# Expert weights loaded from a list of used experts, with experts alternating large and small

## The chip, the cores and the metric

The kernel runs on one core of one Trainium2 chip. The metric is the device time of one execution in microseconds, smaller is better. TensorE (PE in the profile) does the matmuls, VectorE (DVE), ScalarE (ACT) and GpSimd (POOL) the rest, and SyncE (SP) issues most of the transfers. Each engine runs its own program in order and waits on semaphores.

## What is computed

Linear attention (4 batches, 576 tokens, 8 heads of 64), a mixer layer over tokens and channels, and then a layer of experts. Only the last concerns the change. Its core, for the token row `x[b, s]`:

```python
fresh_e = int(np.argmax(logits[b, s]))
if s == 0 or local_gate[b, s] < 0.5:
    e = fresh_e
else:
    e = prev_e if prev_e >= 0 else fresh_e
...
h = np.maximum(x[b, s] @ w1[e], 0.0)
out[b, s] = p[e] * (h @ w2[e])
```

There are 8 experts (`E`), each with `w1[e]` of 512x1024 and `w2[e]` of 1024x512 in float32, 4 MB together. How many tokens fall on an expert depends on the data. Evaluating the reference on this input gives, for experts 0 to 7, 0, 0, 0, 835, 973, 5, 88 and 403 tokens, which is 7, 8, 1, 1 and 4 tiles of 128 rows for experts 3 to 7, 21 tiles in all. In the first three batches alone the counts of experts 3 to 7 are 809, 806, 2, 88 and 23.

## The kernel before

**Stages.** The first part (attention and mixer) goes batch by batch. While the last batch is in its 32 channel chunks, `route_early(idx)` does small pieces of the routing of the first three batches between chunks: at `idx == 13` the counts of the experts are in `bank[3]`, and `order_experts` picks the expert with the most tokens (`expert0`). The others follow it cyclically by number (`expert_at`). Its weights are loaded at once, and the first `EARLY = 3` tiles are filled from the first three batches. The full routing of all tokens (`slots_of_lanes` and what follows) runs on DVE beside tiles 0 to 2. `ids` (row numbers of the tokens of each tile) and `table` (expert, version and so on of each tile) come out of it.

**A tile.** For tile t, POOL gathers 128 token rows into `xg` (`gather`), PE transposes them (`x_turn`), computes the hidden layer in two halves of 512 (`hidden`), transposes it (`h_turn`), multiplies by `w2` (`output`), DVE scales it (`yo_out`), and POOL scatters the rows to the output. PE's order within tile t from tile 3 on is:

```python
h_turn(t, 0, again)
hidden(t, n, 1, again)
x_turn(t + 1)
output(t, n, 0, again)
h_turn(t, 1, again)
next_n = version_of(t + 1)
hidden(t + 1, next_n, 0, again=True)
output(t, n, 1, again)
```

Each float32 weight is split into a high and a low part: ACT writes the high part, DVE the low part, both reading `w1raw` or `w2raw`. A set of weights has 8 units of 512 KB: 0 to 3 are `w1`, 4 to 7 are `w2`. The raw buffer holds one set, the split form two (slots `n & 1`). A set is called a version: version n is the n-th expert loaded.

**When weights are split.** `plan_loads` writes `plan`: an expert's second tile splits `w1` of the next version, its third tile splits `w2` of it; an expert with only one tile has to do both in that tile. For the first expert, tile 3 counts as the second tile. ACT and DVE do the splits between their other work of the tile, in program order.

**When weights are loaded.** SP waits for `routed >= 2` (tables and row numbers both written), then walks over the tiles from 1 on. For each it loads `table` entries into registers (lines 449, 439, 440), and where the tile begins a new expert it loads the 8 units, each behind a wait that the previous version's unit is split (`w_split`). The last of the eight positions counts as a change even if no tile belongs to it (`is_last`), so a set is also loaded behind the last tile.

Of the kernel before, what the change touches and what calls it, by code (L numbers as in the profile page):

```python
# [22 lines left out]
ALU = mybir.AluOpType  # L23
# [6 lines left out]
P = 128  # L30
# [6 lines left out]
def build(nc, q, k, v, w_tok1, w_tok2, w_ch1, w_ch2, w_gate, w_local, w1, w2, out):  # L37
# [42 lines left out]
    with ExitStack() as ctx:  # L80
# [14 lines left out]
        is_last = sb(ctx, "is_last", [1, E])  # L95
# [4 lines left out]
        expert_at = sb(ctx, "expert_at", [P, 2, E], I32)  # L100
        code_at = sb(ctx, "code_at", [P, E])
        token = sb(ctx, "token", [P, J])
# [45 lines left out]
        with ExitStack() as part2:  # L148
# [24 lines left out]
            table = sb(part2, "table", [1, 5, NTP], I32)  # L173
# [34 lines left out]
            expf = sb(part2, "expf", [1, NTP + 1])  # L208
            expert0 = sb(part2, "expert0", [1, 1])
            changes = sb(part2, "changes", [1, NTP + 1])  # L210
# [5 lines left out]
            tg = sb(part2, "tg", [1, NTP, E - 1])  # L216
            tw = sb(part2, "tw", [1, NTP, E - 1])
            starts = sb(part2, "starts", [1, E])
            expi = sb(part2, "expi", [1, NTP], I32)
# [32 lines left out]
        xg_cleared, order_known = sem("xg_cleared"), sem("order_known")  # L252
        own_counted, counts_ready, sel_counted, base_ready = sem("own_counted"), sem("counts_ready"), sem("sel_counted"), sem("base_ready")
# [73 lines left out]
        def _(sp):  # L327
# [92 lines left out]
            e = sp.value_load(expert_at[0:1, 1, 0:1], min_val=0, max_val=E - 1)  # L420
# [17 lines left out]
            def load_weights(t):  # L438
                e = sp.value_load(table[0:1, 0, bass.ds(t, 1)], min_val=0, max_val=E - 1)
                changed = sp.value_load(table[0:1, 1, bass.ds(t, 1)], min_val=0, max_val=1)  # L440
                with sp.If(changed):
                    before = sp.value_load(table[0:1, 4, bass.ds(t, 1)], min_val=0, max_val=E)
# [12 lines left out]
        def _(pe):  # L455
# [267 lines left out]
            def version_of(t):  # L723
                return pe.value_load(table[0:1, 2, bass.ds(t, 1)], min_val=0, max_val=E)
# [68 lines left out]
            with pe.Fori(EARLY, NT) as t:  # L793
                live = pe.value_load(table[0:1, 3, bass.ds(t + 1, 1)], min_val=0, max_val=1)
                with pe.If(live):
                    tile(t, again=True)
# [3 lines left out]
        def _(act):  # L800
# [219 lines left out]
            with act.Fori(EARLY, NT) as t:  # L1020
                live = act.value_load(table[0:1, 3, bass.ds(t + 1, 1)], min_val=0, max_val=1)
                with act.If(live):
                    tile(t, again=True)
# [3 lines left out]
        def _(dve):  # L1027
# [105 lines left out]
            def clear_routing():  # L1133

                beside(dve.memset(expf[:, 0:1], 0.0))
                beside(dve.memset(changes[:, 0:1], 0.0))
# [73 lines left out]
            def order_experts():  # L1210

                assert E & (E - 1) == 0
# [477 lines left out]
```

## Time and profile before

| | us |
|---|---|
| median of 3 runs | 794.91 (794.33 to 796.45) |
| profiled execution, its own time | 790.27 |
| its span in the profile | 788.6 |
| PE busy in the span | 749.5 (95%) |

The times that follow are read from the profiled execution, from the start of its span. Its first part lasts to about 487 us, the tiles of the experts fill the rest. A tile can be followed by PE's rows: L641 is `x_turn`, L718 `output`, L705 `h_turn`, L693 `hidden`. The start of `output(t, 0)` of tile t stands at 539.14 us for tile 3, 560.27 for 4, 609.73 for 8, 622.10 for 9, 696.29 for 15, 712.93 for 16, 729.80 for 17 and 742.39 for 18. The distance between two such starts is called a pitch here.

### The profile page before, as it was taken

What the parts mean: (1) busy time and instruction counts of PE and PEld (TensorE: products, weight loads), DVE (VectorE), ACT (ScalarE), POOL (GpSimd) and SP (SyncE); (2) the same over time, 40 slices, a digit from 0 to 9 for tenths busy, and PEclk for the clock granted to TensorE, in tenths of its full rate; (3) what the DMA queues carried; (4) which work ended last, traced back from release to release, by engine and by line L of the source; (5) the groups of instructions that cost most, each with busy time, mean ns of one, the idle gap of its engine ahead of it and who ended that gap; (6) DMA issues with size and microseconds to landing.
All of it is one profiled execution on the core that took longest, in us unless ns stands there. A gap on an engine that the chain in (4) does not pass through costs nothing.

```text
span 788.6 us, 14829 instructions
## 1 busy us (share of the span) xinstructions
PE 749.5 (95%) x4836; PEld 678.5 (86%) x4837; DVE 316.6 (40%) x611; ACT 234.1 (30%) x409; POOL 142.4 (18%) x162
## 2 busy tenths in 40 slices
PE   6999999999999999999999999996999999997993
PEld 6879999999999999999999999874888888875882
DVE  6746241225332235332225424762522622257450
ACT  3743042023132023133021141313422522255340
POOL 6562020002020002020000023111221221211220
PEclk9999999999999999999999999999999999999998
DMA  9932122012131012100010510105360620136400
GB/s 210 378 66 59 33 68 54 1 32 61 31 81 41 1 32 62 31 21 11 1 35 1 196 62 16 62 28 190 118 230 34 211 90 26 36 134 210 155 27 2
DMA packets 69514, 61.80 MB, mean 78 GB/s; under 512 B 51484, under 2 KB 53244, under 8 KB 69472
## 3 DMA queue, kind: packets, MB, share of 16 engines
q1 hardware_dynamic: 65952, 51.77, 22.2%
q0 software_dynamic: 3520, 9.44, 3.5%
q8 instruction: 30, 0.49, 0.3%
q14 instruction: 12, 0.10, 0.0%
HBM read 52.99 MB, written 10.31 MB: 80 GB/s over the span
## 4 chain that ended last, share of the span: by engine, by line
PE 80%; DVE 6%; issue 3%; DMA 3%; POOL 2%; ACT 2%; SPq 2%; DVEq 1%; ACTq 0%; POOLq 0%
PE bank L572 36%; PE bank L718 13%; PE bank L693 12%; PE bank L514 5%; PE bank L543 4%; POOL qb L1577 2%; PE bank L705 2%; PE bank L537 2%; PE bank L486 2%; DMA x_rows<-x1n 1%; PE bank L593 1%; PE bank L502 1%; PE bank L582 1%; PE bank L524 1%; PE bank L641 1%
## 5 line engine op out<-in xcount | busy, mean ns | idle before, releaser
L572 PE MATMUL bank<-u_h,wc_h 128*128 128x288 f32 x384 | 120.0, 312 | 1.5 <-DVE hid_l L1303 1.5
L718 PE MATMUL bank<-wslots,hT_h 128*128 (+1 forms) x336 | 107.5, 401 | 10.1 <-DVE hT_l L1470 10.1
L572 PE MATMUL bank<-hid_h,wc_h 128*128 128x288 f32 x384 | 117.0, 305 | 0.0
L693 PE MATMUL bank<-wslots,xgT_h 128*128 (+1 forms) x344 | 111.8, 406 | 4.2 <-DVE wslots L1454 3.1
L572 PE MATMUL bank<-hid_l,wc_h 128*128 128x288 f32 x384 | 113.2, 295 | 0.0
L572 PE MATMUL bank<-u_l,wc_h 128*128 128x288 f32 x384 | 113.1, 295 | 0.0
L572 PE MATMUL bank<-u_h,wc_l 128*128 128x288 f32 x384 | 113.0, 294 | 0.0
L572 PE MATMUL bank<-hid_h,wc_l 128*128 128x288 f32 x384 | 113.0, 294 | 0.0
L1303 DVE SCALAR_TENSOR_TENSOR hid_l<-bank,hid_h 128x288 fp32r<-128x288 f32 x96 | 43.3, 454 | 132.4 <-ACT hid_h L872 132.2
L718 PEld LDWEIGHTS bank<-wslots,hT_h 128*128 128x128 f32 x336 | 62.1, 191 | 23.5 <-issue 10.8
L693 PEld LDWEIGHTS bank<-wslots,xgT_h 128*128 128x128 f32 x344 | 61.0, 188 | 17.9 <-issue 7.0
L872 ACT ACTIVATE hid_h<-bank 128x288 fp32r<-128x288 f32 x96 | 38.9, 408 | 123.4 <-PE bank L572 123.4
L572 PEld LDWEIGHTS bank<-u_h,wc_h 128*128 128x128 f32 x384 | 72.1, 188 | 2.9 <-DVE hid_l L1303 1.8
L572 PEld LDWEIGHTS bank<-u_l,wc_h 128*128 128x128 f32 x384 | 72.2, 188 | 0.7
L572 PEld LDWEIGHTS bank<-hid_l,wc_h 128*128 128x128 f32 x384 | 72.2, 188 | 0.5
L572 PEld LDWEIGHTS bank<-hid_h,wc_h 128*128 128x128 f32 x384 | 72.0, 188 | 0.6
L572 PEld LDWEIGHTS bank<-hid_h,wc_l 128*128 128x128 f32 x384 | 72.3, 188 | 0.0
L572 PEld LDWEIGHTS bank<-u_h,wc_l 128*128 128x128 f32 x384 | 72.0, 188 | 0.0
L693 PE MATMUL bank<-wslots,xgT_l 128*128 (+1 forms) x172 | 67.4, 392 | 0.0
L718 PE MATMUL bank<-wslots,hT_l 128*128 (+1 forms) x168 | 66.3, 394 | 0.0
L1310 DVE TENSOR_TENSOR x1T<-bank,u_h 128x288 f32<-128x288 f32 x32 | 14.6, 457 | 117.2 <-PE bank L572 117.2
L1577 POOL TENSOR_TENSOR qb<-qb,qmax 96x768 f32<-96x768 f32 x12 | 17.6, 1471 | 231.2 <-DVE qmax L1072 231.2
(236 smaller groups left out, 1090.2 us busy)
## 6 DMA issues: line engine op xcount, KB each, us to landing
w1raw<-in_moe_w_dram SPq DMA_DIRECT2D x24, 512.0 KB, 4.6
w2raw<-in_moe_w_dram SPq DMA_DIRECT2D x24, 512.0 KB, 6.4
wc_raw<-in_moe_w_ch_dram SPq DMA_DIRECT2D x8, 768.0 KB, 11.2
x_rows<-x1n SPq DMA_DIRECT2D x24, 192.0 KB, 2.1
kb<-in_k_dram SPq DMA_DIRECT2D x24, 144.0 KB, 3.1
qb<-in_q_dram SPq DMA_DIRECT2D x24, 144.0 KB, 3.1
vb_e<-in_v_dram SPq DMA_DIRECT2D x16, 144.0 KB, 3.6
vb_o<-in_v_dram SPq DMA_DIRECT2D x16, 144.0 KB, 3.4
```

The source lines that it names most:

```text
L486: last = pe.matmul(k_bank(n, g)[:, c * KV:(c + 1) * KV], keys(n)[:, i, c * P:(c + 1) * P], vb[g][:, 2 * c:2 * c + 2, i, :], start=(i == 0) ...
L514: last = pe.matmul(mix_bank(n, g)[:, c * TOK:(c + 1) * TOK], queries(n)[:, i, c * P:(c + 1) * P], wt1[:, i, :], start=(i == 0), stop=(i == ...
L537: pe.matmul(bank[4 + j % 2][:, 0:HS], kvd[:, c // CG, c % CG, :], qT[:, c // CG, c % CG, part], start=True, stop=False)
L543: last = pe.matmul(bank[4 + j % 2][:, 0:HS], h1T[:, m, c * P:(c + 1) * P], wt2[:, m, part], start=False, stop=(m == KT - 1))
L572: last = pe.matmul(to, lhsT, rhs, start=(m == 0), stop=(m == len(mms) - 1))
L693: last = pe.matmul(bank[half][:, :], xgT[a][:, c, :], w1s[x][:, bass.ds(n & 1, 1), c, half * 512:(half + 1) * 512].rearrange("p a n -> p ( ...
L705: last = pe.transpose(bank[2 + half][:, c * P:(c + 1) * P], hs[:, f * P:(f + 1) * P], ident[:, :])
L718: last = pe.matmul(bank[5][:, :], hT[a][:, f, :], w2s[x][:, bass.ds(n & 1, 1), f, :].rearrange("p a n -> p (a n)"), start=(f == 0 and (a, ...
L872: act.activation(hid[0][:, i, :], bank[idx % 2][:, 0:HS], ACT.Relu).then_inc(hid_hi, 1)
L1303: dve.scalar_tensor_tensor(out=hid[1][:, i, :], in0=psum, scalar=0.0, in1=hid[0][:, i, :], op0=ALU.max, op1=ALU.subtract).then_inc(chan_do ...
L1310: dve.tensor_tensor(x1T[:, i, :], psum, u[0][:, i, part], ALU.add).then_inc(y_sum, 1)
L1577: pool.tensor_tensor(by_head(queries(n))[:, IHALF[part], :, :], x[:, IHALF[part], :, :], by[:, IHALF[part], :].unsqueeze(3).broadcast_to([ ...
```

## The change

Three things are done. (1) `order_experts` only finds the first expert; a new `place_experts`, run on DVE at `idx == 15`, ranks all experts by their count in the first three batches and places ranks 0, 1, 2, ... of the asked-for experts alternately from the large and the small end. (2) A new `versions`, on DVE ahead of `yo_out(1)`, writes a list `loads` of the experts that have tiles; SP waits for it (`versions_known`) and loads set after set from the list, with no walk over tiles and no set for an expert without tiles. (3) On DVE `ids_out` comes ahead of `tables`; POOL waits only for the row numbers before it gathers tile 3; PE does the first half of `output(2, ..., 1)` ahead of `x_turn(3)`.

```diff
             def order_experts():
-                then(dve.tensor_scalar(expert_at[:, 0, :], lane[:, 0:E], top0[:, E + 1:E + 2], float(E), ALU.subtract, ALU.add))
-                then(dve.tensor_scalar(expert_at[:, 1, :], expert_at[:, 0, :], E - 1, None, ALU.bitwise_and))
-                beside(dve.tensor_copy(expert0[:, :], expert_at[0:1, 1, 0:1]))
-                then(dve.tensor_scalar(code_at[:, :], expert_at[:, 1, :], -1.0, float(E), ALU.mult, ALU.add), order_known)
+                then(dve.tensor_scalar(expert0[:, :], top0[0:1, E + 1:E + 2], -1.0, float(E), ALU.mult, ALU.add), order_known)
+
+            def place_experts():
+
+                beside(dve.scalar_tensor_tensor(out=key[:, :], in0=bank[3][:, 0:E], scalar=float(E), in1=code[:, :], op0=ALU.mult, op1=ALU.add))
+                then(dve.tensor_scalar(asked[:, :], bank[3][:, 0:E], 0.0, None, ALU.is_gt))
+                beside(dve.tensor_reduce(twice[:, 0:1], asked[:, :], AX_X, ALU.add))
...
+                then(dve.tensor_reduce(rank[:, :], over_key[:, :, :], AX_X, ALU.add))
+                then(dve.tensor_scalar(up[:, :], rank[:, :], 2.0, None, ALU.mult))
+                then(dve.scalar_tensor_tensor(out=down[:, :], in0=up[:, :], scalar=-1.0, in1=twice[:, 1:2].broadcast_to([P, E]), op0=ALU.mult, op1=ALU.add))
+                beside(dve.scalar_tensor_tensor(out=place[:, :], in0=down[:, :], scalar=0.0, in1=rank[:, :], op0=ALU.is_lt, op1=ALU.mult))
+                then(dve.tensor_tensor(up[:, :], up[:, :], down[:, :], ALU.min))
+                then(dve.tensor_tensor(place[:, :], place[:, :], up[:, :], ALU.max))
...
@@ SP @@
-            sp.wait_ge(routed, 2)
-            with sp.Fori(1, NT + 1) as t:
-                go = sp.value_load(table[0:1, 3, bass.ds(t, 1)], min_val=0, max_val=1)
-                with sp.If(go):
-                    load_weights(t)
+            def load_weights(n):
+
+                e = sp.value_load(loads[0:1, 0, n:n + 1], min_val=0, max_val=E - 1)
+                asked_for = sp.value_load(loads[0:1, 1, n:n + 1], min_val=0, max_val=1)
+                with sp.If(asked_for):
                     for i in range(NU):
-                        sp.wait_ge(w_split, NU * before + i + 1)
+                        sp.wait_ge(w_split, NU * (n - 1) + i + 1)
                         load_unit(e, i)
+            sp.wait_ge(versions_known, 1)
+            for n in range(1, E):
+                load_weights(n)
@@ PE @@
             output(2, 0, 0, True, SECOND)
+            output(2, 0, 1, True, FIRST)
             x_turn(EARLY)
-            output(2, 0, 1, True)
-            pe.wait_ge(routed, 1)
+            output(2, 0, 1, True, SECOND)
+            pe.wait_ge(routed, 2)
@@ DVE @@
             row_lanes(P, rowhot, rows_hot)
+            versions()
             yo_out(1, True)
 
             hT_out(2, 0)
+            ids_out()
             tables()
-            ids_out()
             plan_loads()
@@ POOL @@
-                    pool.wait_ge(routed, 2)
+                    pool.wait_ge(routed, 1)
```

`versions` is nine small operations on one partition (the last writes `loads` and signals `versions_known`); `tables` has 7 in place of 13.

On SP, behind its last stores of token rows, stood the walk over tiles. These are its first rows, one pass up to the branch that skips a tile without a new expert; the loads of the units follow that branch:

```order
L448 UNCONDITIONAL_BRANCH [waits routed]
L448 ISA
L449 TENSOR_LOAD table
L449 ISA x2
L450 COMPARE_AND_BRANCH
L439 ISA
L439 TENSOR_LOAD table
L439 ISA x2
L440 ISA
L440 TENSOR_LOAD table
L440 ISA x2
L441 COMPARE_AND_BRANCH
```

At the same place of SP now stands the first entry of the list, with the first unit of the weights right behind it:

```order
L451 TENSOR_LOAD loads [waits versions_known]
L451 ISA x2
L452 TENSOR_LOAD loads
L452 ISA x2
L453 COMPARE_AND_BRANCH
L381 ISA [waits w_split]
L381 DMA w1raw<-in_moe_w_dram 128x1024
```

The walk is gone: two register loads stand between the wait and the first transfer, where each pass of the walk has three.

On DVE, beside tile 2, the end of `tables` (L1409 to L1417) stood ahead of the row numbers `ids` (`ids_out`, L1422 to L1424); `yo_out(1)` and `hT_out(2, 0)` stand ahead of both:

```order
L1409 CAST tiles<-first_tile 1x1
L1411 TENSOR_SCALAR expi<-expf,expert 1x29
L1412 TENSOR_SCALAR table<-expi 1x29 [waits route]
L1413 CAST table<-changes 1x29
L1414 CAST table<-changes 1x29
L1415 TENSOR_TENSOR changed<-expf 1x29
L1416 TENSOR_SCALAR table<-lane,first_tile 1x29
L1417 CAST table<-changed 1x29 [waits route]
L1422 COPY prob_t<-bank 128x24 [waits ids_ready,route,routed]
L1423 TENSOR_SCALAR ids<-bank 128x24
L1424 TENSOR_TENSOR prob_t<-prob_t,bank 128x24 [waits route,routed]
```

Now the end of `versions` (L1438, L1439) comes ahead of `yo_out(1)` (L1514), and the row numbers ahead of `tables` (L1443 on):

```order
L1438 TENSOR_REDUCE loads_f<-by_version 1x8 [waits route]
L1439 CAST loads<-loads_f 1x8 [waits route]
L1514 TENSOR_SCALAR yo<-bank,prob_t 128x512 [waits y_ready,rows_stored,route,versions_known]
L1503 TENSOR_TENSOR hT_l<-bank,hT_h 128x512 [waits hT_hi]
L1455 COPY prob_t<-bank 128x24 [waits ids_ready]
L1456 TENSOR_SCALAR ids<-bank 128x24
L1457 TENSOR_TENSOR prob_t<-prob_t,bank 128x24 [waits route,routed]
L1443 TENSOR_TENSOR tg<-lane,first_tile 1x232 [waits route]
L1446 TENSOR_REDUCE begun<-tg 1x29 [waits route]
```

`ids` moved ahead of the tables, and the nine operations of `versions` ahead of the scaling of tile 1.

On PE, at the end of tile 2, `x_turn(3)` (L641) stood between the two halves of `output(2)`:

```order
L718 MATMUL bank<-wslots,hT_h 128x512 x2
L718 MATMUL bank<-wslots,hT_l 128x512
L641 MATMUL bank<-ident,xg 128x128 [waits x_in]
L641 MATMUL bank<-ident,xg 128x128 x3
L718 MATMUL bank<-wslots,hT_h 128x512 [waits w_split,hT_done]
L718 MATMUL bank<-wslots,hT_h 128x512
```

Now six matmuls of the second half stand ahead of it:

```order
L727 MATMUL bank<-wslots,hT_h 128x512 [waits w_split,hT_done]
L727 MATMUL bank<-wslots,hT_h 128x512
L727 MATMUL bank<-wslots,hT_l 128x512
L727 MATMUL bank<-wslots,hT_h 128x512 x2
L727 MATMUL bank<-wslots,hT_l 128x512
L650 MATMUL bank<-ident,xg 128x128 [waits x_in]
L650 MATMUL bank<-ident,xg 128x128 x3
```

PE's wait for the gathered rows (`x_in`) moved behind those six.

## Rows read from the trace of the kernel before

**Rows 1.** Stretches: length, busy of PE, PEld, DVE, ACT, POOL, granted clock, DMA share, GB/s.
```profile
539.14:560.27 21.13, 14.48 (x64) 11.56 (x63) 7.45 (x8) 7.03 (x10) 2.44 (x4) 0.84 0.60 214
...
609.73:622.10 12.37, 12.37 (x62) 10.19 (x61) 7.46 (x8) 6.68 (x10) 3.15 (x4) 1.00 0.63 213
...
696.29:712.93 16.64, 13.50 (x61) 9.72 (x60) 11.91 (x12) 11.96 (x17) 2.12 (x3) 1.00 0.63 219
712.93:729.80 16.87, 13.46 (x61) 9.96 (x61) 11.90 (x12) 9.40 (x13) 3.06 (x4) 1.00 0.57 190
729.80:742.39 12.59, 12.59 (x61) 10.47 (x62) 2.82 (x4) 2.20 (x4) 3.49 (x5) 1.00 0.56 216
```

**Rows 2.** Timeline of PE in tile 3: start, length, instruction, idle before and its releaser.
```profile
551.99 1.22 PE L718 MATMUL bank<-wslots,hT_h 128*128 x2 [6.65 <-DVE hT_l L1470]
```

**Rows 3.** The chain that ended last, in order of time: start, length, what.
```profile
524.08 0.29 SPq L449
...
542.47 0.37 SPq L370
543.12 5.41 DMA w1raw<-in_moe_w_dram
...
551.99 4.64 PE bank L718 x12
...
560.27 2.77 PE bank L718 x12
```

**Rows 4.** Timeline of DVE beside tiles 1 and 2.
```profile
516.21 2.69 DVE L1202 TENSOR_TENSOR rowhot<-sloti,lane 128x768 fp32r<-128x768 int32 x3
519.40 0.75 DVE L1481 TENSOR_SCALAR yo<-bank,prob_t 128x512 f32<-128x512 f32 x1 [0.51 <-PE bank L718]
...
521.07 0.14 DVE L1403 SCALAR_TENSOR_TENSOR starts<-ntl,is_last 1x8 f32<-1x8 f32 x1
...
523.40 0.17 DVE L1417 CAST table<-changed 1x29 int32<-1x29 f32 x1
...
523.71 0.17 DVE L1423 TENSOR_SCALAR ids<-bank 128x24 int32<-128x24 f32 x1
```

**Rows 5.** Timeline of POOL, PE and DVE around x_turn(3).
```profile
525.16 1.06 POOL L1613 DMA_INDIRECT xg<-x_rows,id_in  x1 [0.87 <-POOL id_in L1610]
...
528.65 0.66 PE L641 MATMUL bank<-ident,xg 128*128 128x128 f32 x4 [0.88 <-DMA xg<-x_rows,id_in]
...
529.98 0.69 DVE L1294 TENSOR_TENSOR xgT_l<-bank,xgT_h 128x512 fp32r<-128x512 f32 x1 [2.14 <-ACT xgT_h L909]
...
531.88 0.61 PE L693 MATMUL bank<-wslots,xgT_h 128*128 x2
```

**Rows 6.** DMA issues between 570 and 576 us: count, KB, median us to landing.
```profile
out_dram<-yo,id_out POOLq DMA_INDIRECT x1, 7.5
xg<-x_rows,id_in POOLq DMA_INDIRECT x1, 6.0
```

**Rows 7.** DMA issues between 445 and 452 us.
```profile
xg<-x_rows,id_in POOLq DMA_INDIRECT x1, 7.6
```

**Rows 8.** Timeline of DVE and PE behind chunk 15 of the last batch.
```profile
442.55 0.46 DVE L1303 SCALAR_TENSOR_TENSOR hid_l<-bank,hid_h 128x288 fp32r<-128x288 f32 x1 [0.57 <-ACT hid_h L872]
...
447.88 0.38 PE L572 MATMUL bank<-u_h,wc_h 128*128 128x288 f32 x1
```

**Rows 9.** Timeline of SP and POOL around those transfers.
```profile
446.97 1.92 SPq L374 DMA_DIRECT2D w2raw<-in_moe_w_dram  x4
448.76 1.23 POOL L1613 DMA_INDIRECT xg<-x_rows,id_in  x1 [0.98 <-POOL id_in L1610]
...
568.38 2.10 SPq L370 DMA_DIRECT2D w1raw<-in_moe_w_dram  x4
570.67 2.77 SPq L374 DMA_DIRECT2D w2raw<-in_moe_w_dram  x4
```

**Rows 10.** The stretch in which the later of those two sets landed, columns as in Rows 1.
```profile
568.38:583.00 14.62, 14.62 (x73) 12.07 (x72) 3.79 (x6) 3.48 (x6) 2.44 (x4) 1.00 0.90 322
```

More of the change, by code:

```diff
@@ L99, in build @@
         top0 = sb(ctx, "top0", [P, E + 2])
-        expert_at = sb(ctx, "expert_at", [P, 2, E], I32)
+        expert_at = sb(ctx, "expert_at", [P, E])
+        expert0 = sb(ctx, "expert0", [1, 1], I32)
         code_at = sb(ctx, "code_at", [P, E])
+        key = sb(ctx, "key", [P, E])
+        over_key = sb(ctx, "over_key", [P, E, E])
+        rank = sb(ctx, "rank", [P, E])
+        asked = sb(ctx, "asked", [P, E])
+        twice = sb(ctx, "twice", [P, 2])
+        up = sb(ctx, "up", [P, E])
+        down = sb(ctx, "down", [P, E])
+        place = sb(ctx, "place", [P, E])
         token = sb(ctx, "token", [P, J])
@@ L170, in build @@
             id_out = sb(part2, "id_out", [P, 1], I32)
[L173 removed]
+            table = sb(part2, "table", [1, 2, NTP], I32)
             plan = sb(part2, "plan", [1, 4, NTP], I32)
@@ L215, in build @@
             slots = sb(part2, "slots", [P, J, E])
[L216 to L219, printed above, removed]
+            tg = sb(part2, "tg", [1, NTP, E])
+            used = sb(part2, "used", [1, E])
+            used_before = sb(part2, "used_before", [1, E + 1, E])
+            version_at = sb(part2, "version_at", [1, E + 1])
+            named = sb(part2, "named", [1, E])
+            by_version = sb(part2, "by_version", [1, E, E])
+            loads_f = sb(part2, "loads_f", [1, E])
+            loads = sb(part2, "loads", [1, 2, E], I32)
             yo = sb(part2, "yo", [P, D])
@@ L252, in build @@
         xg_cleared, order_known = sem("xg_cleared"), sem("order_known")
+        versions_known = sem("versions_known")
         own_counted, counts_ready, sel_counted, base_ready = sem("own_counted"), sem("counts_ready"), sem("sel_counted"), sem("base_ready")
@@ L419, in _ @@
             sp.wait_ge(order_known, 1)
-            e = sp.value_load(expert_at[0:1, 1, 0:1], min_val=0, max_val=E - 1)
+            e = sp.value_load(expert0[0:1, 0:1], min_val=0, max_val=E - 1)
             for i in range(FU):
@@ L1286, in route_early @@
                     early_lanes()
+                elif idx == 15:
+                    place_experts()
                 elif idx == 17:
@@ new lines, in versions @@
+            def versions():
+                then(dve.tensor_scalar(used[:, :], ntl[0:1, :], 0.0, None, ALU.is_gt))
+                beside(dve.tensor_tensor(used_before[:, :, :], used[:, :].unsqueeze(1).broadcast_to([1, E + 1, E]), below[0:1, :, :], ALU.mult))
+                then(dve.tensor_tensor(named[:, :], used[:, :], expert_at[0:1, :], ALU.mult))
+                then(dve.tensor_reduce(version_at[:, :], used_before[:, :, :], AX_X, ALU.add))
+                beside(dve.tensor_scalar(loads[:, 1, :], lane[0:1, 0:E], version_at[:, E:E + 1], None, ALU.is_lt))
+                then(dve.tensor_tensor(by_version[:, :, :], version_at[:, 0:E].unsqueeze(1).broadcast_to([1, E, E]),
+                                       lane[0:1, 0:E].unsqueeze(2).broadcast_to([1, E, E]), ALU.is_equal))
+                then(dve.tensor_tensor(by_version[:, :, :], by_version[:, :, :], named[:, :].unsqueeze(1).broadcast_to([1, E, E]), ALU.mult))
+                then(dve.tensor_reduce(loads_f[:, :], by_version[:, :, :], AX_X, ALU.add))
+                then(dve.tensor_copy(loads[:, 0, :], loads_f[:, :]), versions_known)
@@ L1433, in plan_loads @@
                 beside(dve.tensor_tensor(only, now, ahead, ALU.mult))
-                beside(dve.tensor_scalar(more, changes[:, 1:NTP + 1], changes[:, NTP:NTP + 1], None, ALU.is_lt))
-                then(dve.tensor_scalar(plan[:, 3, :], changes[:, 1:NTP + 1], 1.0, None, ALU.add))
+                beside(dve.tensor_scalar(more, begun[:, 1:NTP + 1], begun[:, NTP:NTP + 1], None, ALU.is_lt))
+                then(dve.tensor_copy(plan[:, 3, :], begun[:, 1:NTP + 1]))
                 beside(dve.scalar_tensor_tensor(out=later, in0=now, scalar=0.0, in1=more, op0=ALU.is_equal, op1=ALU.mult))
```

55 lines of the change are left out of this document (23 added, 32 removed).

## Prediction

> **What bounds the kernel now.** I read the page first: PE is busy 95% of the span, so only places where PE stands still can give time back, or places where it would newly stand still. The change touches the stage of the experts, so next I cut that stage at each start of `output(t, 0)` and read the pitches [rows 1]. An undisturbed tile takes 12.37 us, and that includes a tile in which ACT and DVE split the four `w1` units of the next expert: the stretch of tile 8 has 7.46 us of DVE work and PE is still busy for all of its 12.37 [rows 1]. So a split costs nothing if its raw weights are there. Three stretches are longer, and one slightly.
>
> Tile 3 to tile 4 takes 21.13 us, 8.76 too many. The reader is to see PE idle for 6.65 us behind DVE's `hT_l` [rows 2], and a granted clock of 0.84 of full speed in that stretch where others have 1.00 [rows 1]; the twelve matmuls behind the idle time took 4.64 us where the same twelve take 2.77 [rows 3]. The chain of waits says what is late: SP starts its walk over the tiles at 524.08 and issues the first load of the next expert at 542.47, after seven passes of 2.6 us each; the unit lands 5.4 us later, ACT and DVE split, and only then does DVE come to `hT_out(3, 1)` [rows 3]. The wait is for SP's walk, not for bandwidth.
>
> Tiles 15 and 16 take 16.64 and 16.87 us, and the tile after them 12.59 [rows 1]. These are the two experts with one tile each: DVE has 11.9 us of work in each, since all eight units are split in one tile. The three excesses are 4.27, 4.50 and 0.22, together 8.99 us.
>
> **The order of the experts.** The counts of the first three batches rank the experts 3, 4, 6, 7, 5 (809, 806, 88, 23, 2 tokens). Five are asked for, so `twice` is 9; `up` is twice the rank and `down` is 9 less that. The smaller of the two is the place: 0, 2, 4, 3, 1. The order is 3, 5, 4, 7, 6, with 7, 1, 8, 4 and 1 tiles, where it was 3, 4, 5, 6, 7 with 7, 8, 1, 1 and 4. Tile 7 now belongs to expert 5 alone, tile 20 to expert 6 alone. Tile 7 has another expert behind it and has to split both parts of it. Tile 20 has none behind it, since the new tables count no expert without tiles, and its own weights are split in tiles 17 and 18, the second and third of expert 7. So one tile with eight splits is left of two.
>
> **Its price.** Tile 7 is what tile 15 was: the raw weights were loaded tiles before, and the next expert is needed at once. I give it tile 15's excess of 4.27 and the 0.22 of the tile behind [rows 1], 4.49 us. Gone is the other one: 8.99 less 4.49 is **4.5 us gained**. The set behind the last tile goes too, with its eight splits on ACT and DVE in tiles 18 and 19; by tile 8 such splits lie under PE's work [rows 1], so this gives nothing.
>
> **The wait in tile 3.** `versions` has nine small operations behind `row_lanes`, which ends at 518.90 (516.21 + 2.69). The thirteen operations of the old tables, some with 203 columns, went from 521.07 to 523.57, 0.19 us each [rows 4]; nine at this price are 1.7 us, so the list is known at about 520.6. SP then needs two register loads and a branch, half of a 2.6 us pass [rows 3], and issues its first unit at about 522.0, 20 us earlier than before. ACT wanted the units from about 540 on. The set issued from 568.38 on was 4.19 MB in a stretch that moved 322 GB/s [rows 9, 10], 13 us; even at 190 GB/s, the lowest rate of a stretch with such loads [rows 1], it is 22 us, and the `w1` half is in by 533. Tile 3 then looks like tile 8, splits with no waits: 21.13 less 12.37, **8.8 us gained**, the slow clock included.
>
> **What the early load does to the gather of tile 3.** This is what goes the other way. Before, the loads began behind this gather; now they begin ahead of it. `yo_out(1)` waits for `versions` and moves from 519.40 to about 520.7. The row numbers no longer stand behind the tables, so they come about 1.4 us earlier than the 523.71 of before [rows 4] (520.7, plus 0.7 for `yo_out`, 0.7 for `hT_out(2, 0)`, 0.2), and POOL's gather moves from 525.16 [rows 5] to about 523.75. On an idle queue it landed 3.4 us after its issue: PE's transpose began at 528.65, 0.88 us late [rows 5]. With loads in flight such transfers took longer. A scatter and a gather issued between 570 and 576 us, behind a set of loads that began at 568.38, landed after 7.5 and 6.0 us [rows 6, 9], and a gather 1.8 us behind the first of four loads after 7.6 [rows 7, 9]. The new gather stands 1.75 us behind the first load, so the last is the nearest, and I take 7.6: the rows are there at 531.35. PE reaches the transpose at 529.2 (527.77 in the old trace, and the six matmuls moved ahead of it, half of a 2.77 us group [rows 3]), so it waits 2.2 us. From transpose to the next `hidden` the old trace has 2.05 us through ACT and DVE (528.65 to 529.98 + 0.69 [rows 5]); with 0.1 us to notice the rows, `hidden(3)` starts 2.15 us after the landing, at 533.5 where it was 531.88 [rows 5]: **1.6 us lost**. Bounds: at 6.0 us nothing is lost, at 3.4 the moved matmuls win 0.5 us.
>
> The gather of tile 4 is issued as PE ends that transpose, at about 533.2, and is wanted at 540.4; 7.2 us are just about enough.
>
> The Trainium skill, "DMA: Bandwidth & Descriptors", section "Queues, rings and completion order", says that each DMA engine takes turns between its queues packet by packet. By that rule a gather shares with the loads and does not stand behind all of them; if sharing doubled its 3.4 us, it would land at 530.6 and the loss would be 0.8, the sum 0.8 us better. The trace agrees that it is not strictly behind: the 7.6 and 6.0 us stand against the 13 us of a whole set.
>
> **What lies under other work.** `place_experts` has fifteen operations, 2.9 us at the same 0.19, behind chunk 15 on DVE. Waiting behind it are the low parts of chunk 16, before at 442.55, now about 445.0. PE wants them for chunk 18, which began at 447.88 [rows 8], since the early row sums and the logits lie between. The margin is 2.4 us; without it the cost would be the part over. `tables` now ends about 0.9 us later than before, but PE wants it only at `hidden(3)`, 7 us on. POOL and the loop bodies are as before.
>
> **The sum.** -8.8 - 4.5 + 1.6 = -11.7 us. Against the profiled execution: 790.27 gives 778.6, a span of 776.9. That execution is 4.6 us below the median of the runs shown, 794.91; I carry the difference over: 783.2 us. With the gather's bounds it is 781.1 to 783.3, and with one microsecond for what I cannot see, 780.0 to 784.5.
>
> **The rivals.**
> (a) One-tile tiles still cost twice. If the ranks came out so that both single experts have another behind them, nothing is gained there: -8.8 + 1.6 = -7.2, 787.7. For it: 809 against 806 is close. Against: exchanging those two leaves the small experts where they are, and 88, 23, 2 are far apart. Likewise if tile 7 costs a second 4.5. 8%.
> (b) The gather stands behind the whole set of loads, at 322 GB/s [rows 10]: it lands 13 us after 522.0, at 535.0; `hidden(3)` starts 5.3 us late, and PE's slower clock after such idle time costs another 1.9, as it did in tile 3 (4.64 less 2.77 [rows 3]). -13.3 + 7.2 = -6.1, 788.8. Against it stand the 7.6 and 6.0 us. 6%.
> (c) The same, but the set moves at 190 GB/s as in tile 16's stretch [rows 1]: 22.1 us, landing at 544.1, 14.4 us late, and 1.9 for the clock. -13.3 + 16.3 = +3.0, **slower**, 797.9. It decides from a landing at 541.1, 19 us after the first load, which is 220 GB/s for the set. The stretches at 213 and 219 GB/s [rows 1] are short of loads, not of rate, since one set did 322. 3%.
> (d) The change doesn't do what it says: the list comes no earlier than the walk did, because `versions_known` is delayed by something ahead of it on DVE. Then little is gained in tile 3, -4.5 at best, 790.4. For it speaks nothing in the timeline of DVE, which is not idle there but in time. 3%.
> (e) More is gained than I count, for instance the small waits around tile 3 too: -14.5, 780.4 or a little under. 8%.
> The forecast, -10.5 to -14, has 72%.
>
> **How the numbers follow.** The range holds the forecast and (a) and most of (e): 780.0 to 788.0, leaving out (b), (c), (d). A measurement tells 0.3%, 2.4 us, from no change. Faster by more than that are all but (c) and a rest of unknown things: 0.95 faster, 0.02 the same, 0.03 slower.
>
> **What would show it.** In the new profile: SP's first load behind the first set at about 522; no idle time of PE behind `hT_l` in tile 3 and a pitch near 12.4 there; gather 3 landing 6 to 8 us after its issue, and PE's transpose waiting about 2 us; one stretch of about 16.6 us at tile 7, none at tiles 15 and 16; five sets of loads, 20 `w1` units; chunk 18 of the last batch not waiting for DVE. I would be wrong if tile 3 keeps a wait for weights, if tile 7 costs more than tile 15 did, or if the gather lands after more than 10 us.

## The result, and the profile after

The changed kernel took 782.34 us, the median of 4 runs (780.17 to 785.64), against 794.93 us of the kernel before (794.33 to 796.45, 4 runs on the same chip). The ratio is 0.9846, with a 95% interval of 0.9814 to 0.9878: 12.6 us less, where 11.7 were forecast.

The profiled execution took 782.87 us, with a span of 781.1. I cut it at the starts of `output(t, 0)` as [rows 1] were: tiles 3, 5, 7, 8, and the stretch from `x_turn(20)` to the end.

```profile
545.62:557.92 12.30, 12.30 (x63) 10.11 (x62) 7.46 (x8) 6.78 (x10) 3.23 (x4) 1.00 0.58 191
570.24:582.57 12.33, 12.33 (x64) 10.18 (x62) 2.82 (x4) 2.89 (x6) 2.46 (x4) 1.00 0.06 22
594.86:611.78 16.92, 13.79 (x64) 9.99 (x62) 11.90 (x12) 11.28 (x15) 2.12 (x3) 1.00 0.65 212
611.78:624.08 12.30, 12.30 (x60) 10.21 (x61) 2.83 (x4) 1.95 (x4) 3.48 (x5) 1.00 0.31 105
759.14:781.10 21.96, 9.27 (x45) 7.40 (x43) 2.13 (x3) 2.28 (x4) 2.46 (x4) 0.80 0.03 10
```

The first row is to be held against the first of [rows 1]: tile 3 holds its four splits of `w1` still (7.46 us of DVE, where a plain tile has 2.82), yet PE is busy in all of its 12.30 us, the clock is 1.00, and 8.83 us are gone. The third row, with 11.90 us of DVE, is the one expensive tile that is left.

The timelines of SP, DVE, POOL and PE around `x_turn(3)` show the list, the loads and the gather (start, length, instruction, idle before and its releaser).

```profile
525.32 0.16 DVE L1439 CAST loads<-loads_f 1x8 int32<-1x8 f32 x1
526.87 0.17 DVE L1456 TENSOR_SCALAR ids<-bank 128x24 int32<-128x24 f32 x1
...
526.88 1.96 SPq L381 DMA_DIRECT2D w1raw<-in_moe_w_dram  x4
...
528.33 1.06 POOL L1645 DMA_INDIRECT xg<-x_rows,id_in  x1 [0.87 <-POOL id_in L1642]
...
535.89 0.66 PE L650 MATMUL bank<-ident,xg 128*128 128x128 f32 x4 [1.50 <-DMA xg<-x_rows,id_in]
...
538.27 0.72 PE L702 MATMUL bank<-wslots,xgT_h 128*128 x2 [0.34 <-DVE xgT_l L1321]
```

This trace runs 4.90 us behind the one of before when `hidden(0)` begins (492.04 against 487.14), so 4.9 is to be taken off each time before it is compared. The first load then stands at 522.0, 20 us earlier than in [rows 3]. The gather is issued 1.45 us behind it, lands 7.52 us later, and PE waits 1.50 us for it, where it waited 0.88 in [rows 5] with no load in flight. From the issue of the gather to `hidden(3)` are 9.94 us, before 6.72.

The whole difference between the two traces, stretch by stretch:

| stretch | before | after | difference |
|---|---|---|---|
| start to `hidden(0)` | 487.14 | 492.04 | +4.90 |
| to `hidden(3)` | 44.74 | 46.23 | +1.49 |
| to `output(3, 0)` | 7.26 | 7.35 | +0.09 |
| tile 3 | 21.13 | 12.30 | -8.83 |
| the one-tile tiles and the one behind, over plain tiles | 8.99 | 4.60 | -4.39 |
| the rest, 16 plain pitches and the end | | | -0.76 |
| span | 788.6 | 781.1 | -7.5 |

A plain pitch of after is 12.31, the mean of 11 from `x_turn(9)` at 623.73 to `x_turn(20)` at 759.14; the two rows of the one-tile tile and the one behind make 29.22, 4.60 more than two of these. Without the first row of the table the sum is -12.4, near the 12.6 of the medians. The first row is no price of the change as far as 3.6 us go. These had passed when the `w2` loads of the first expert were issued (450.56 against 446.97 [rows 9]), and this trace had a lower granted clock in its first 40 us, where the trace of before had 1.00 in both of these stretches:

```profile
0.00:20.00 20.00, 13.68 (x158) 12.68 (x160) 12.73 (x17) 6.35 (x11) 12.23 (x31) 0.95 1.03 198
20.00:40.00 20.00, 19.55 (x116) 18.22 (x114) 12.45 (x19) 13.47 (x15) 8.90 (x5) 0.88 1.05 365
```

An experiment below with the same code up to there (the load behind the gather) issued those loads at 447.31. The other 1.3 us are a wait of PE between two late chunks, behind `hid_l`, that was 1.54 us and is 2.84; the last experiment takes it up. PE before and after:

```profile
458.54 0.40 PE L572 MATMUL bank<-u_h,wc_h 128*128 128x288 f32 x1 [1.54 <-DVE hid_l L1303]
```

```profile
463.42 0.40 PE L581 MATMUL bank<-u_h,wc_h 128*128 128x288 f32 x1 [2.84 <-DVE hid_l L1330]
```

### The profile page after: what moved, and what is told of

It reads as the page before. It is cut to its first block, busy times and chain, and to the rows that moved or that the text cites. A ratio compares the mean times of both kernels' runs of the same rounds, so it can differ in the third digit from the quotient of the medians.

```text
span 781.1 us, 14381 instructions
## 1 busy us (share of the span) xinstructions
PE 750.2 (96%) x4836; PEld 681.2 (87%) x4837; DVE 309.9 (40%) x617; ACT 226.9 (29%) x401; POOL 141.7 (18%) x160
## 4 chain that ended last, share of the span: by engine, by line
PE 84%; DVE 6%; DMA 3%; POOL 2%; ACT 2%; issue 1%; SPq 0%; DVEq 0%; ACTq 0%; POOLq 0%
PE bank L581 37%; PE bank L702 13%; PE bank L727 13%; PE bank L523 5%; PE bank L552 4%; PE bank L714 2%; POOL qb L1609 2%; PE bank L495 2%; PE bank L546 2%; DMA x_rows<-x1n 1%; PE bank L650 1%; PE bank L511 1%; PE bank L602 1%; PE bank L591 1%; DMA xg<-x_rows,id_in 1%
```

## The experiments

Each ratio is to the kernel before, timed on the same chip as the experiment, with its 95% interval. Unless another kernel is named, the edit is to the changed kernel. The experiments ran on three chips, so differences between the medians of two runs are less sure than the ratios.

**The list alone.** The cyclic order is put back, with everything else kept. Inside `place_experts`:

```diff
-                beside(dve.scalar_tensor_tensor(out=key[:, :], in0=bank[3][:, 0:E], ...
...
-                then(dve.tensor_reduce(expert_at[:, :], over_key[:, :, :], AX_X, ALU.add))
+                then(dve.tensor_scalar(cyclic[:, 0, :], lane[:, 0:E], top0[:, E + 1:E + 2], float(E), ALU.subtract, ALU.add))
+                then(dve.tensor_scalar(cyclic[:, 1, :], cyclic[:, 0, :], E - 1, None, ALU.bitwise_and))
+                then(dve.tensor_copy(expert_at[:, :], cyclic[:, 1, :]))
```

> The changed kernel with its list of loads, but with the experts in the old cyclic order (3, 4, 5, 6, 7). My theory: two separate gains. The tile 3 wait stays gone (pitch of tile 3 near 12.3 us), and the two one-tile experts at tiles 15 and 16 cost again: pitches 16.6, 16.9 and 12.6, together 9 us over three plain tiles, where the changed kernel has 4.6 once. So about 4.5 us slower than the changed kernel, near 787 us, ratio to the kernel before 0.990. Rival: the order has no price of its own, the loads of the walk being late also at tiles 15 and 16; then the pitches there fall to about 14 or less and the time is that of the changed kernel, 782.

787.46 us (786.49 to 788.15), ratio 0.9907 [0.9879, 0.9934]. PE waits in tile 3 no longer; the stretches of tiles 15, 16 and 17 are:

```profile
692.87:709.54 16.67, 13.56 (x61) 9.75 (x60) 11.90 (x12) 11.94 (x17) 2.12 (x3) 1.00 0.63 207
709.54:726.56 17.02, 14.95 (x61) 11.18 (x61) 11.90 (x12) 9.05 (x13) 3.03 (x4) 0.90 0.24 82
726.56:739.15 12.59, 12.59 (x61) 10.47 (x62) 2.82 (x4) 2.68 (x5) 3.50 (x5) 1.00 0.13 42
```

Both expensive tiles are back, as in [rows 1]. By the two ratios the list (with what else the change does to tile 3) is worth 7.4 us (0.0093 of 794.9) and the order 4.9 (0.0061 of it). The second is not all the order: the plain tiles of this run take 12.37 us where the changed kernel's take 12.31, nearly 1 us in all, which the experiment on unused bytes takes up.

**The large experts first, then the small ones.** The place is the rank, so the tiles of the experts are 7, 8, 1, 4, 1.

```diff
-                then(dve.tensor_tensor(place[:, :], place[:, :], up[:, :], ALU.max))
+                then(dve.tensor_copy(place[:, :], rank[:, :]))
```

> The changed kernel with the experts in descending order of count (3, 4, 6, 7, 5 with 7, 8, 1, 4, 1 tiles) instead of large, small, large, small. My theory: what counts is only how many one-tile experts have another expert behind them, here one (tile 15) as in the changed kernel (tile 7). Same time, 782.3 within the noise, ratio 0.985, one pitch of 16.6 us, now at tile 15. Rival (the alternation matters, since a small expert between large ones finds its weights loaded): the single tile costs over 6 us and the time is 785 or more.

781.85 us (780.34 to 782.34), ratio 0.984 [0.9816, 0.9864]: the same as the changed kernel. The expensive pair stands at tiles 15 and 16 now, 15.03 and 14.16 us from one `x_turn` to the next, where the changed kernel has 15.07 and 14.15 for tiles 7 and 8. The alternation as such gives nothing here; what counts is that one of the one-tile experts is the last.

**A set behind the last tile.** One operation makes the last position count as used, so that a sixth set is loaded and split, as the kernel before did.

```diff
+                then(dve.memset(used[:, E - 1:E], 1.0))
```

> The changed kernel, but the eighth position counts as used again, so that a set without tiles is loaded and split behind the last tile, as before the change. My prediction called that set free, because it fell under plain tiles. My theory now: with a one-tile expert last it is not free. Tile 20 must split all eight units; hidden(21) waits 2.3 us for w1 as in the other one-tile tile, and yo_out of tile 20 stands behind four w2 splits on DVE, 3.8 us more. So 6.1 us slower than the changed kernel, near 788.4, ratio 0.992. Rival (the trailing set costs nothing wherever it falls): 782.3, ratio 0.985.

788.29 us (786.61 to 789.72), ratio 0.9921 [0.9896, 0.9947]. The stretch from `x_turn(20)` to the end, and DVE in it:

```profile
758.23:786.30 28.07, 10.34 (x45) 7.26 (x43) 11.31 (x11) 9.85 (x12) 3.15 (x4) 0.80 0.02 8
```

```profile
769.30 4.63 DVE L1488 TENSOR_TENSOR wslots<-w2raw,wslots 128x1024 f32 x4 [3.02 <-ACT wslots L876]
773.85 0.74 DVE L1515 TENSOR_SCALAR yo<-bank,prob_t 128x512 f32<-128x512 f32 x1
```

The stretch has 28.07 us where the changed kernel has 21.96 (last row of its first view above): 6.1 us. PE's last matmul group begins 11.50 us into it (769.73), against 8.88 (768.02), which is 2.6; the other 3.5 stand on DVE, where four splits for an expert that nobody uses come ahead of the last `yo_out`. A one-tile expert in last place is free only since no set follows it.

**The first load later, by two waits.** The first edit lets SP wait for the tables too; the second lets it wait until POOL has asked for the rows of tile 3.

```diff
             sp.wait_ge(versions_known, 1)
+            sp.wait_ge(routed, 2)
```

> The changed kernel, but SP starts on the list only when the tables are written too, about 3.6 us later (first unit near 530.4 on the changed kernel's time axis instead of 526.9). My theory: the gather of tile 3 is issued at 528.3, ahead of the loads, lands after 3.4 to 4.5 us instead of 7.5, and PE's wait of 1.5 us at x_turn(3) goes; w1 is still in before ACT wants it at 546.5. So 1.5 us faster than the changed kernel, 780.8 us, ratio 0.982. Rival (the gather is slow for a reason of POOL's or of its rows, not of the loads): it still takes 7.5 us and the time stays at 782.3.

```diff
             sp.wait_ge(versions_known, 1)
+            sp.wait_ge(rows_asked, EARLY + 1)
```

> The changed kernel, but SP starts on the list when POOL issues the gather of tile 3 (first unit about 1 us behind it, near 529.5). My theory: the gather lands after 3.5 to 5 us, PE waits 0 to 0.3 us at x_turn(3), 780.8 to 781.2 us, ratio 0.982 to 0.983. Rival (what delays a gather is any load in flight beside it, whichever was first): it takes 6 us or more and the gain is under 0.5 us.

They took 780.08 us (778.82 to 782.9), ratio 0.9812 [0.9783, 0.984], and 780.51 us (778.6 to 781.44), ratio 0.9819 [0.9792, 0.9847]. The timelines of the second, POOL, SP and PE:

```profile
525.62 1.06 POOL L1646 DMA_INDIRECT xg<-x_rows,id_in  x1 [0.87 <-POOL id_in L1643]
...
526.27 2.02 SPq L381 DMA_DIRECT2D w1raw<-in_moe_w_dram  x4
...
531.55 0.60 PE L651 MATMUL bank<-ident,xg 128*128 128x128 f32 x4
...
533.86 0.73 PE L703 MATMUL bank<-wslots,xgT_h 128*128 x2 [0.32 <-DVE xgT_l L1322]
```

PE waits for no rows, though the load follows the gather by only 0.65 us; the gather landed after 5.0. With the first edit the load follows by 2.19 us, and the gather landed after 3.3. From its issue to `hidden(3)` are 8.24 us in both, against 9.94. The 1.7 us are the traffic ahead of the gather. That the loads come 2.1 or 3.6 us later costs nothing. The medians fall by 2.3 and 1.8 us, but their intervals overlap that of the changed kernel, so the 1.7 us rest on the traces.

**The first load at the old time, from the list.** SP waits for the tables and then makes seven passes of register loads that load nothing, before it reads the list.

```diff
+            sp.wait_ge(routed, 2)
+            with sp.Fori(1, 8) as t:
+                go = sp.value_load(table[0:1, 1, bass.ds(t, 1)], min_val=0, max_val=1)
+                with sp.If(go):
+                    sp.value_load(table[0:1, 0, bass.ds(t, 1)], min_val=0, max_val=E)
+                    sp.value_load(table[0:1, 1, bass.ds(t, 1)], min_val=0, max_val=1)
```

> The changed kernel with only the delay of the walk put back: SP waits for the tables and then makes seven passes of three register loads, which use nothing, ahead of the list. My theory: the first unit goes out 18 us after the tables, near 547, PE idles 6 to 7 us behind hT_l in tile 3, the clock falls there, and the pitch of tile 3 is 21 us or a little over: 8.8 us lost and 1.5 us at the gather won back, so 7.3 us slower than the changed kernel, near 789.6, ratio 0.993. Rival (the order of DVE's tables and row numbers, or the move on PE, gave the gain of tile 3): the pitch of tile 3 stays under 15 us and the time under 785.

787.77 us (786.81 to 791.26), ratio 0.9915 [0.9884, 0.9946]. SP and PE:

```profile
544.88 2.13 SPq L381 DMA_DIRECT2D w1raw<-in_moe_w_dram  x4
...
554.18 1.22 PE L733 MATMUL bank<-wslots,hT_h 128*128 x2 [5.37 <-DVE hT_l L1509]
```

The idle time of [rows 2] is back, at the same instruction and behind the same releaser, with slow matmuls behind it (1.22 us for two, as there), and tile 3 takes 20.5 us (542.60 to 563.09). The time is a little under the 789.6 forecast, as the load went out at 544.88 and not at 547. So the wait was for the time at which SP issued the load, and the other parts of the change don't remove it.

**The transpose ahead of the matmuls again.** The order of PE around `x_turn(3)` is undone.

```diff
-            output(2, 0, 1, True, FIRST)
             x_turn(EARLY)
-            output(2, 0, 1, True, SECOND)
+            output(2, 0, 1, True)
```

> The changed kernel with PE's order at the end of tile 2 as before the change: x_turn(3) ahead of the whole second half of output(2). My theory: the gathered rows come at the same time, PE waits 1.4 us longer for them (2.9 instead of 1.5), and has all twelve matmuls still to do behind, 2.8 us, which is more than the 2.4 us from transpose to hidden; hidden(3) starts 0.8 us later, 783.1 us. In the profile, 9.9 us from the issue of the gather to hidden(3) become 10.7. Rival (the move gains its whole 1.4 us, or nothing): 11.3 or 9.9 us there.

785.4 us (783.45 to 787.71), ratio 0.9877 [0.9845, 0.9909]. PE's timeline, and the granted clock of the stretch behind the wait:

```profile
536.72 1.11 PE L650 MATMUL bank<-ident,xg 128*128 128x128 f32 x4 [3.44 <-DMA xg<-x_rows,id_in]
537.49 1.20 PE L727 MATMUL bank<-wslots,hT_h 128*128 128x512 f32 x2
```

```profile
536.00:543.00 7.00, 6.28 (x18) 5.13 (x19) 0.86 (x2) 0.60 (x1) 1.43 (x3) 0.54 0.98 376
```

From the gather to `hidden(3)` are 13.7 us in this trace, where I had 10.7 and the changed kernel has 9.94. The wait grew by 1.9 us, and behind it the clock stood at the lower of its two levels, 1.2 GHz, for most of the stretch up to `hidden(3)` (0.54 of full speed in the mean); two matmuls took 1.20 us, 0.62 at full clock. In the changed kernel the clock stayed at 1.00 behind the wait of 1.50 us. From the transpose to `hidden(3)` are 5.9 us here; the kernel before, with the same order and the clock at 1.00, has 3.2 [rows 5]. So 2.7 of the 3.7 us are the clock and 1.0 the order, near my 0.8. The medians differ by 3.1, but the intervals overlap, and the four runs lie in two pairs, 783.5 and 783.7, 787.1 and 787.7; the traced one is of the slower pair. The first pair is near the forecast of 783.1. Whether the clock fell at this place in the slower pair only is not shown, since one run alone has a trace. So the six matmuls moved ahead are worth about what they fill where the clock holds, and more where it falls.

**Place_experts three times.** It gives the same places each time.

```diff
-                    place_experts()
+                    for _ in range(3):
+                        place_experts()
```

> The changed kernel with place_experts done three times in a row, 5.5 us more on DVE at that place. The trace of the changed kernel shows two margins behind it: 3.1 us to chunk 18 on PE, and only 1.4 us idle before hid_l of chunk 17, which early_out follows; on early_out hang the w2 loads, and behind them in SP's queue the token rows that ACT waits for. Theory A: early_out moves by 4.1 us, the stores move with it and PE's wait for them grows from 2.8 to about 4.5, after 2.4 us at chunk 18: 4.1 us slower than the changed kernel, 786.4, ratio 0.990. Theory B (as in my prediction, only chunk 18 counts): 2.4 us slower, 784.7, ratio 0.988.

789.89 us (783.77 to 792.94, 8 runs), ratio 0.9945 [0.9921, 0.9969]. The profiled execution is the fastest of them. PE's waits in it, and two matmuls behind the first of them:

```profile
450.62 0.61 PE L581 MATMUL bank<-u_h,wc_h 128*128 128x288 f32 x1 [2.27 <-DVE hid_l L1331]
...
451.26 0.44 PE L581 MATMUL bank<-u_h,wc_l 128*128 128x288 f32 x1
451.50 0.44 PE L581 MATMUL bank<-u_h,wc_h 128*128 128x288 f32 x1
...
463.29 0.41 PE L581 MATMUL bank<-u_h,wc_h 128*128 128x288 f32 x1 [1.00 <-DVE hid_l L1331]
```

The two further passes are 5.55 us (one is 2.75), and PE waits 2.27 for the low part of chunk 16, so once the placing is done there are 3.3 us to spare. I had 2.4. From the first `w1` load to `hidden(0)` this trace has 3.2 us more than the changed kernel's. The two waits together are only 0.4 longer: the second, which theory A let grow to 4.5, fell from 2.84 to 1.00. The other 2.8 us are the clock, which neither theory had: behind the 2.27 us it stood at 0.50 for 5.4 us, with matmuls 0.24 us apart instead of 0.133. The median has 7.5 more. Six of the other seven runs have a lower mean clock (down to 0.978, the profiled one 0.988), which would fit a clock that falls in more places; without traces of those runs this stays open.

**Unused bytes in SBUF.** Plain tiles take 12.31 us, and took 12.37 [rows 1], with the same instructions in them. The edit puts 64 unused bytes ahead of other tiles on each partition.

```diff
+        sb(ctx, "unused", [P, 2, E], I32)
```

> The changed kernel with 64 bytes of each SBUF partition set aside and not used, so that every tile allocated behind them lies 64 bytes further. The plain tiles of the changed kernel have a mean pitch of 12.31 us, those of the kernel before and of the run with the cyclic order 12.37; the latter has just such 64 bytes more. Theory A (the addresses of the operands decide it): the mean pitch is 12.37 us here, 1.0 us more over the tiles from 3 on. Theory B (the order or the instruction stream decides it): it stays 12.31.

782.05 us (781.0 to 784.71), ratio 0.9836 [0.9809, 0.9863]. A plain tile:

```profile
583.34:595.71 12.37, 12.37 (x62) 10.19 (x61) 2.83 (x4) 2.88 (x5) 2.47 (x4) 1.00 0.13 42
```

It takes 12.37 us again, while the time is as it was: 0.06 us in each of some 16 tiles is 1 us, less than this measurement can tell. So where the operands lie moves the pitch. That the kernel before has its 12.37 us for the same reason is likely but not shown; if so, this part of the changed kernel's gain is an accident of its allocation.

**Two attempts at the tile that is left.** Both build on the load behind the gather. Two of the eight splits of a one-tile expert move into the tile behind it; ACT and DVE each need two more register loads per tile for that.

```diff
+            def late_units(t):
+                late = act.value_load(plan[0:1, 2, bass.ds(t - 1, 1)], min_val=0, max_val=1)
+                n = act.value_load(plan[0:1, 3, bass.ds(t - 1, 1)], min_val=0, max_val=E)
+                with act.If(late):
+                    for i in (6, 7):
+                        unit_hi(n, i, n & 1)
...
-                units(t + 1, weights, 2, (4, 5, 6, 7), again)
+                units(t + 1, weights, 2, (4, 5), again)
```

> The version with the loads behind the gather of tile 3, and in addition the last two w2 splits of a one-tile expert moved behind the first hT_out of the next tile on ACT and DVE. My theory: of the 4.3 us that tile 7 costs, 2.3 are the wait of hidden for w1 and stay, and 1.9 are hT_out(8, 0) standing behind four w2 splits; these two splits fewer take 2.4 us off DVE there, so the pitch of tile 7 falls from 16.6 to about 14.8, and nothing else moves. 778.7 us, ratio 0.980. Rival (the split work itself is the limit, wherever it stands): the wait comes back at output(8, 1) or hidden of the next tile, pitches 7 and 8 together stay at 29.2, and the time is 780.5.

793.94 us (791.97 to 795.1, 12 runs), ratio 0.9998 [0.9984, 1.0012]. The timeline of ACT in a plain tile:

```profile
665.99 0.60 ACT L991 ACTIVATE hs<-bank 128x512 f32<-128x512 f32 x1 [3.45 <-issue]
```

ACT stands 3.45 us before `hs_out` with nothing to wait for but its own instructions that the profile doesn't count, and every plain tile takes 12.75 to 12.92 us. The six tiles that split `w1` or `w2` beside others (second and third tiles) suffer more, 13.44 to 13.96 us. So the forecast of 778.7 missed by 15 us, and the rival's 780.5 too. The second attempt does the late splits behind `xgT_out` instead:

```diff
-                late_units(t)
                 weights = next_weights(t)
                 hs_out(t, 1)
                 xgT_out(t + 1)
+                late_units(t)
```

> As the run with late w2 splits, but with the two late splits, and the two register loads that decide on them, behind xgT_out on ACT and DVE instead of ahead of it. In the last run two more register loads ahead of hs_out held up hs, xgT_h and so hidden of the next tile, 0.5 us in every tile. Theory A: behind xgT_out they are under PE's output and cost nothing; plain tiles are 12.31 us again, tile 7 about 14.8 instead of 16.6. 778.7 us, ratio 0.980. Rival (two register loads cost each tile wherever they stand, or the split work is the limit): plain tiles over 12.5 us, or tiles 7 and 8 together 29.2 us or more, and 780.5 or slower.

789.12 us (786.12 to 789.73), ratio 0.9916 [0.9892, 0.9941]. ACT and PE in tile 7:

```profile
596.76 2.01 ACT L877 ACTIVATE wslots<-w1raw 128x1024 f32 x2 [1.17 <-issue]
...
599.55 0.73 PE L703 MATMUL bank<-wslots,xgT_h 128*128 x2 [1.46 <-DVE wslots L1496]
```

Plain tiles are at 12.31 again, but the register loads stand ahead of the splits that PE wants at once: the pair from one `x_turn` to the next takes 18.17 and 13.23 us where it took 15.07 and 14.15, 2.2 more. The larger part is in the six tiles with splits, which take 13.34 to 13.59 us, 7.1 more together; in the first two of them ACT stands 1.04 and 1.23 us before its first split. Neither is worth having.

**The row stores ahead of `w2`.** Between chunks ACT copies token rows into `x1n`, two buffers, and SP stores them. The edit, on top of the load behind the gather, puts the first two of these stores ahead of the first expert's `w2` loads.

```diff
+            for i in range(HI - 1):
+                store_rows(LAST, i)
             sp.wait_ge(early_ids, 1)
             for i in range(FU, NU):
                 load_unit(e, i)
-            for i in range(HI):
-                store_rows(LAST, i)
+            store_rows(LAST, HI - 1)
```

> The changed kernel with the first weight load behind the gather (e3), and on SP's queue the first two row stores of the last batch go out ahead of the w2 loads of the first expert, the third behind them. Theory: in the changed kernel those stores stand behind w2's loads, land in 8 to 9.4 us, and PE's wait behind the last chunk (2.84 us at 463.42 in its profile) stands in that shadow; with the stores first they land 2 to 4 us after their issue, the wait falls by 1.5 to 2.8 us and w2 is still in before ScalarE wants it at about 476. Against e3's 780.5 that gives 778.2 us, 0.979 of the kernel before. Rival: the wait is ended by something else (the rows of x themselves, or hidden work on VectorE, which is named as its releaser), and the time stays at 780.5, 0.982.

776.83 us (774.8 to 777.89), ratio 0.9778 [0.9759, 0.9797], the fastest kernel here. First the timelines of SP, ACT and PE in the kernel without this edit, and the stretch behind the wait:

```profile
449.28 9.41 SPq L369 DMA_DIRECT2D x_rows<-x1n  x3
...
457.77 0.59 ACT L866 ACTIVATE x1n<-bank 96x512 f32<-96x512 f32 x1 [3.62 <-DMA x_rows<-x1n]
...
459.21 0.40 PE L582 MATMUL bank<-u_h,wc_h 128*128 128x288 f32 x1 [1.88 <-DVE hid_l L1331]
...
461.46 0.45 PE L582 MATMUL bank<-u_l,wc_h 128*128 128x288 f32 x1
461.70 0.45 PE L582 MATMUL bank<-u_h,wc_l 128*128 128x288 f32 x1
...
464.03 0.29 PE L582 MATMUL bank<-u_h,wc_h 128*128 128x288 f32 x1
464.16 0.29 PE L582 MATMUL bank<-u_l,wc_h 128*128 128x288 f32 x1
```

```profile
459.00:465.00 6.00, 5.79 (x32) 5.79 (x33) 1.30 (x4) 0.82 (x2) 0.00 (x0) 0.72 0.11 33
```

And ACT with it, behind SP's first two stores:

```profile
450.73 2.37 SPq L369 DMA_DIRECT2D x_rows<-x1n  x2
...
455.78 0.59 ACT L867 ACTIVATE x1n<-bank 96x512 f32<-96x512 f32 x1
```

The chain is: the first store lands late behind the weights (ACT's wait for it ends 8.1 us after its issue before the change, 9.4 in the changed kernel, 8.5 here), ACT waits for the buffer (4.59 us there), the high parts of the next chunks stand behind its copy, DVE's low parts behind these, and PE behind DVE. The page names DVE, but a transfer is late. With the edit ACT writes the third copy 5.05 us after the issue of the first store and doesn't wait, so that store had landed by then; the three land after 5.4 us in the median, where they took 7.0 (I had 2 to 4). PE's wait is gone. More came back than the wait: behind the 1.88 us the clock fell, and fourteen matmuls in a row began 0.24 us apart instead of 0.133, which is 1.5 us. From the first `w1` load to `hidden(0)` are 51.9 us with the edit and were 55.6, 3.7 less, and the medians differ by 3.7 too. But the clock doesn't fall there in every execution (last section), the two kernels ran on different chips, and their intervals overlap a little, so the size is less sure than the cause.

## Why the prediction was right

The terms came out one by one, as follows. That the total agrees within 0.9 us is in part luck. In the traces of the changed kernel and the experiments the first `w1` load of the first expert, up to which all have the same code, goes out between 433.67 and 439.79 us, by the clock of the first 40 us; and the losses by the row stores and by the clock, below, were in no term.

**The wait in tile 3**: -8.76 forecast, -8.83 measured. The list came with 9 operations in 1.8 us (1.7 forecast), the first load at 522.0 on the old axis, as forecast. That its time alone made the wait is shown by its return when SP was made late again.

**The order**: -4.50 forecast, -4.39 measured. Tile 7 and the one behind cost 4.60 where tile 15 cost 4.49, and no second tile does, where rival (a) had two. The prediction said that the set behind the last tile gives nothing by going. Beside plain tiles that holds; under the new order it would have cost 6.1 us, more than the whole gain of the order, which hangs on its absence.

**The gather**: +1.6 forecast, +1.49 measured, by a landing time of 7.52 us against 7.6 taken from [rows 7], and PE waited 1.50 where I had 2.2. On the old axis the rows were asked for at 523.43 rather than 523.75, and PE reached the transpose 0.3 us later than I had it. What asking for the rows 1.7 us earlier (525.16 before) is worth by itself was not tried. That the traffic ahead of the gather does it is shown by the two later loads, with which 1.7 us are back. Rivals (b) and (c), a gather behind the whole set, fell with that landing. By the rule of the Trainium skill, "DMA: Bandwidth & Descriptors", section "Queues, rings and completion order", the gather takes turns with the loads. The trace agrees, since 7.52 us are far less than the 13 us that the 4.19 MB of the set take at the 321 GB/s of that stretch. The doubling of 3.4 to 6.8 us that I weighed beside it was too little.

**What was missed.** The fall of the clock behind short waits was in no term for the early load; undoing the move of the matmuls cost 3.7 us in its trace, 2.7 of them by the clock. Plain tiles became 0.06 us shorter, which no step foresaw. The wait for the row stores of the last batch stands in the trace of before already (1.54 us), and I didn't look at it; taking it away in a kernel with the new list gave some 3.7 us, 1.5 of them by the clock. In the eleven traces of kernels with the new list, the placing done once and the stores behind `w2`, it is 1.79 to 2.92 us; whether the change lengthened it, one trace of before can't tell. **Place_experts** lay under other work, with a little more room than I gave it (3.3 us, I had 2.4).

## What to carry to other kernels

A loop that finds the next transfer by walking over a table costs its whole walk before the first byte moves; write the list of what is needed where it is computed, and let the queue read that. Then look at what stands right behind the new transfer: a small transfer on which an engine waits belongs ahead of the large one, and 0.65 us ahead were enough here. Where an engine's idle time is put down to another compute engine, follow that engine's own waits until a transfer or a queue is reached.

## What the runs showed of the hardware that I had not expected

- The granted clock falls behind some short waits of PE, and not by their length alone. At one place, PE's wait between the late chunks, twelve traces can be compared. The clock fell behind waits of 1.79 (cyclic order), 1.88 (load behind the gather, and late splits), 2.56 (transpose first) and 2.92 us (unused bytes). It stayed at 1.00 behind 1.54 (before), 1.81, 1.85, 2.12, 2.22, 2.33 and 2.84 us (changed kernel). From the first `w1` load to `hidden(0)`, less the wait, are 53.7 us in the five with the fall and 52.2 in the six others with the new list. So such a wait can cost its length alone or 1.5 us more, from one execution to the next.
- A gather of 128 rows took 3.3 to 3.4 us with no load issued within 2 us of it, 5.0 us with four loads issued from 0.65 us behind it, and 7.52 with the first 1.45 us ahead of it.
- The pitch of a tile of the same matmuls is 12.31 or 12.37 us, by where its operands lie in SBUF.
- Two more register loads and a branch in each tile on ACT and DVE, ahead of `hs_out`, cost 0.44 to 0.61 us of each plain tile and 1.1 to 1.6 us of the tiles with splits. Behind `xgT_out` they cost plain tiles nothing and the tiles with splits 1.0 to 1.3 us.
